# Seven products for the four blocks of the first layers, weights streamed, the low parts of the weights' four sums on VectorE

## The reference

```python
attn_out = _attn_ref(q, k, v)                       # rotate q and k, softmax(q k^T / 8) v
x = attn_out.transpose(0, 2, 1, 3).reshape(2304, 512)
h = x @ w_in;  r = np.maximum(h, 0.0);  x = (s * (r * r) + b) @ w_out              # MLP 1
h = x @ w2_in; g = h * (1.0 / (1.0 + np.exp(-1.702 * h)));  return g @ w2_out      # MLP 2
```

## Time and profile before

| what | value |
|---|---|
| runs | 1119.51, 1119.0, 1119.11 us; median 1119.11 us |
| profiled execution, span from its first to its last instruction | 1117.4 us |
| granted TensorE clock, mean | 0.998 |
| busy: PE, VectorE, ScalarE, GpSimd | 98%, 50%, 45%, 22% |
| matmuls of the first layers (L956) | 2304 of 128x384 |
| matmuls of the second layers (L984) | 1152 of 128x384, 864 of 128x512 |

### The profile page before, as it was taken

How to read it: one execution, slowest core, us unless ns; L and a number is a source line. 1 busy time by engine, 2 the same in 40 slices (tenths; PEclk the granted TensorE clock), 3 DMA queues, 4 the chain that set the end, 5 groups by cost and what they waited for, 6 DMA issues and landing times.

```text
span 1117.4 us, 16936 instructions
## 1 busy us (share of the span) xinstructions
PE 1090.4 (98%) x6522; PEld 1036.1 (93%) x6522; DVE 553.5 (50%) x885; ACT 500.8 (45%) x1031; POOL 247.4 (22%) x276
## 2 busy tenths in 40 slices
PE   4899999999999999999999999999999999999998
PEld 4899999999999999999999999999999999999997
DVE  6888888898866333333333356532332323333222
ACT  4888788878755332232332345422322222222222
POOL 6878878895720000000000000000000000000000
PEclk9999999999999999999999999999999999999999
DMA  4555454553243100000000014200000000000000
GB/s 109 126 147 145 128 152 130 147 138 91 69 132 125 37 1 1 1 1 1 1 1 1 1 57 133 76 1 1 29 1 29 1 15 15 1 29 1 29 1 29
DMA packets 59187, 59.47 MB, mean 53 GB/s; under 512 B 13780, under 2 KB 46820, under 8 KB 59108
## 3 DMA queue, kind: packets, MB, share of 16 engines
q1 hardware_dynamic: 58272, 57.90, 18.6%
q10 hardware_dynamic: 836, 0.49, 0.1%
HBM read 35.88 MB, written 4.79 MB: 36 GB/s over the span
## 4 chain that ended last, share of the span: by engine, by line
PE 90%; DVE 4%; ACT 3%; DMA 1%; issue 1%; POOL 1%; SPq 0%; ACTq 0%; POOLq 0%; DVEq 0%
PE psum L956 36%; PE psum L984 36%; PE psum L651 7%; PE psum L605 4%; PE psum L579 4%; ACT E L713 2%; DVE negmax L805 1%; PE psum L681 1%; DVE osum L835 1%; DVE Xlo L815 1%; PE psum L615 0%; PE psum L631 0%; DMA sin<-in_k_sin_dram 0%; PE psum L679 0%; DVE QK L858 0%
## 5 line engine op out<-in xcount | busy, mean ns | idle before, releaser
L956 PE MATMUL psum<-xhi,Wlo 128*128 128x384 f32 x768 | 257.8, 336 | 0.0
L956 PE MATMUL psum<-xhi,Whi 128*128 128x384 f32 x768 | 257.6, 335 | 0.0
L956 PE MATMUL psum<-xlo,Whi 128*128 128x384 f32 x768 | 257.2, 335 | 0.0
L956 PEld LDWEIGHTS psum<-xhi,Whi 128*128 128x128 f32 x768 | 144.2, 188 | 4.2
L956 PEld LDWEIGHTS psum<-xlo,Whi 128*128 128x128 f32 x768 | 144.1, 188 | 4.1
L956 PEld LDWEIGHTS psum<-xhi,Wlo 128*128 128x128 f32 x768 | 144.1, 188 | 0.0
L937 DVE SCALAR_TENSOR_TENSOR glo<-act,sb_sb,ghi 128x384 fp32r<-128x384 f32 x96 | 59.4, 619 | 145.4 <-ACT ghi L924 145.4
L924 ACT ACTIVATE ghi<-act,sb_sb 128x384 fp32r<-128x384 f32 x96 | 59.2, 617 | 157.7 <-PE psum L984 150.3
L940 DVE TENSOR_TENSOR glo<-act,ghi 128x384 fp32r<-128x384 f32 x96 | 53.6, 559 | 152.0 <-ACT ghi L926 152.0
L984 PE MATMUL psum<-ghi,Whi 128*128 128x384 f32 x384 | 128.3, 334 | 0.0
L984 PE MATMUL psum<-glo,Whi 128*128 128x384 f32 x384 | 128.3, 334 | 0.0
(11 more groups left out here) (107 smaller groups left out, 1844.4 us busy)
## 6 DMA issues: line engine op xcount, KB each, us to landing
Q<-QK SPq DMA_DIRECT2D x60, 144.0 KB, 3.1
QK<-QK SPq DMA_DIRECT2D x30, 288.0 KB, 3.4
wraw<-in_moe_w_in_dram SPq DMA_DIRECT2D x32, 256.0 KB, 2.9
wraw<-in_moe_w_out_dram SPq DMA_DIRECT2D x32, 256.0 KB, 3.1
vraw<-in_v_dram SPq DMA_DIRECT2D x32, 128.0 KB, 2.3
raw<-in_q_dram SPq DMA_DIRECT2D x30, 128.0 KB, 2.9
raw<-in_k_dram SPq DMA_DIRECT2D x30, 128.0 KB, 2.8
inv_row<-inv_dram SPq DMA_DIRECT2D x16, 144.0 KB, 2.9
```

What stands on the lines that cost most here:

```text
L956: mm = pe.matmul(hps(n), w[i][:, kt * P:(kt + 1) * P], x[C % 2][:, kt, :], start=kt == 0 and j == 0, stop=kt == KT - 1 and j == 2)
```

## The change

`H_step`, `Y_step`, `gate`, `extras`, `load_weights`, `split_w` and `first_w` are taken out. The MLPs now go by chunks of 768 tokens (3 for each MLP) and in a chunk by 8 **windows** of 256 columns of d_ff, 48 windows in all. A window's first layer is a 2 by 2 block product (two blocks of 128 d_ff columns, `a` and `b`, by two blocks of N = 384 tokens; d_model in two halves of 2 slices). It is made of 7 block products in place of 8, each of 2 slices by 3 matmuls of 128x384: `product(pe, n, k)`, k = 0 to 6. For them x has the four sums T1 to T4, made by GpSimd (`x_sum`), and the weights the four sums S1 to S4, made by GpSimd too (`w_sum`). Only two PSUM banks are there for the products: 0, 2, 4, 6 go to one, 1, 3, 5 to the other; products 0, 1 and 3 start a bank afresh, the others add to it; so ScalarE or VectorE has to read a bank out between one product and the next in it. Both layers' weights are loaded and split again in each chunk, into two buffers. The outputs of the second layer add up in the six other banks, in one set. The buffers of x are single.

What each engine issues in window n (768, 1024, ... are elements in each partition):

- PE: product 0, second layer of window n-2, block b, part 0; product 1, part 1; product 2, part 2; product 3, second layer of window n-1, block a, part 0; product 4, part 1; product 5, part 2; product 6. In MLP 1 the pieces of a block are of 512, 256, 256, 512 columns twice, in MLP 2 six of 512, with 3 matmuls each.
- ScalarE: `act_window`, VectorE: `dve_window`, GpSimd: `pool_window`, SP: the loop at the end of the diff.

```diff
-    CH = 384
+    N = 384
+    CH = 2 * N
+    W_OF = (0, 1, 4, 3, 5, 6, 2)
+    NOPS = 7
+    FRESH = (0, 1, 3)
+    POOL_OPS = 2
-    ... gate@-2 ... icp@-1 hi10@-1 hi11@-1 hi12@-1 hi13@-1 xhi@-8 split@-1 evac0@-1 ...          (ACT_ORDER)
+    ... first@-2 ... icp@-1 hi10@-1 hi11@-1 hi12@-1 hi13@-1 xc02@-1 xc03@-1 wsplit@-1 xc04@-1 evac0@-1 xc05@-1 xc06@-1 ...
-    ... lo01@0 split@-1 gate@-1 sum1@-1 ... lo13@0 max00@2 sum0@0 max01@2 ...                    (DVE_ORDER)
+    ... lo01@0 first@-1 sum1@-1 ... lo13@0 max00@2 xc02@0 xc03@0 xc04@0 sum0@0 xc05@0 xc06@0 max01@2 ...
-    POOL_ORDER = order("rot1@3 eps@0 V0@0 V1@0 vlo0@0 vlo1@0 finish@-1 xlo@-9 rot0@4")
+    POOL_ORDER = order("rot1@3 eps@0 V0@0 V1@0 vlo0@0 vlo1@0 finish@-1 rot0@4")
@@ attention_gpsimd @@
+                def first_x(k):
+                    pool.tensor_tensor(xc_hi[k][:], x_source(0, k), zero..., ALU.add).then_inc(first_x_hi, 1)
+                    pool.tensor_tensor(xc_lo[k][:], x_source(0, k), xc_hi[k][:]..., ALU.subtract).then_inc(first_x_lo, 1)
                 def after(s):
-                    first_w(pool, s, zero)
+                    if s == NPAIR - 4:
+                        for step in range(4):
+                            x_sum(pool, 0, step)
+                    if s == NPAIR - 3:
+                        first_w_sums()
+                        first_w_hi()
+                    if s == NPAIR - 2:
+                        win_low(pool, 0)
+                        first_x(0)
+                    if s == NPAIR - 1:
+                        first_x(1)
+                        w_sum(pool, 1)
@@ attention_tensor, first_H @@
-                        H_step(pe, 0)
+                        product(pe, 0, 0)
+                        product(pe, 0, 1)
@@ attention_scalar: xc is x_high (xc_hi[k], 768), wsplit is second_w (win_high(act, 1)), first is keep_first(act, 0) @@
@@ attention_vector: xc is x_low (xc_lo[k], 768), first is block_11(dve, 0) @@
+            def w_sum(pool, m):
+                pool.wait_ge(win_in[m % 2], 48 * (m // 2 + 1))
+                need(pool, win_lo_done, m)
+                need(pool, sums_lo_done, m - 1)
+                pool.tensor_tensor(S1, a21, a22, ALU.add).then_inc(w_sum_step, 1)
+                pool.tensor_tensor(S3, a11, a21, ALU.subtract)
+                pool.tensor_tensor(S2, S1, a11, ALU.subtract).then_inc(w_sum_step, 1)
+                pool.tensor_tensor(S4, a12, S2, ALU.subtract).then_inc(w_sums, 1)
+            def win_high(act, m):
+                act.wait_ge(w_sums, m + 1)
+                need(act, product_done, 7 * (m - 1))
+                act.copy(win_hi[m % 2][:, 0:3 * BLK], win_raw[m % 2][:, 0:3 * BLK])
+                act.copy(win_hi[m % 2][:, 3 * BLK:7 * BLK], wsum[:]).then_inc(win_hi_done, 1)
+            def win_low(pool, m):
+                if m == 0:
+                    sums_low(pool, m)
+                pool.tensor_tensor(win_lo[m % 2][:, 0:3 * BLK], ...[0:3 * BLK], ALU.subtract).then_inc(win_lo_done, 1)
+            def sums_low(eng, m):
+                eng.wait_ge(win_hi_done, m + 1)
+                last = eng.tensor_tensor(win_lo[m % 2][:, 3 * BLK:7 * BLK], wsum[:], win_hi[...], ALU.subtract)
+            def product(pe, n, k):
+                if k == 0:
+                    pe.wait_ge(win_lo_done, n + 1)
+                    need(pe, sums_lo_done, n)
+                if j == 0: (wait for xc_lo of product k)
+                k 0: dve_read 3n; 1: act_read 4n (MLP 2: last_read too); 2: act_read 4n+1; 3: dve_read 3n+1;
+                k 4: act_read 4n+2; 5: act_read 4n+3; 6: dve_read 3n+2
+                for t in range(HK):
+                    for i, (w, x) in enumerate(((win_hi, xc_hi), (win_hi, xc_lo), (win_lo, xc_hi))):
+                        mm = pe.matmul(hps(n, k), w[n % 2][:, at:at + P], x[k][:, t, :], ...)
+            def act_window(act, n):            (in this order; splits: last window of a chunk, evacuates: second)
+                a_b[:, 0:N] <- bank of product 6 of n-1; ga_hi <- a_a (768, waits sq_a)
+                P1 <- bank (product 0); j == 0: xc_hi[6]; splits: xc_hi[0]; win_high(act, n + 1)
+                gb_hi <- a_b (768); splits: xc_hi[1]; evacuates: bank 0
+                U2 <- bank (product 2); splits: xc_hi[2]; evacuates: banks 2, 4; wout_high(act, n) (1024)
+                P5 <- bank (product 3); splits: xc_hi[3], xc_hi[4]; a_b[:, N:] <- h_b; splits: xc_hi[5]; a_a <- h_a (768)
+            def dve_window(dve, n):
+                a_a, a_b squared or multiplied (768 each); ga_lo (768); j == 0: xc_lo[6]; splits: xc_lo[0]; evacuates: bank 1
+                block_11: h_a[:, 0:N] <- bank (product 1) + P1; sums_low(dve, n + 1) (1024)
+                gb_lo (768); evacuates: banks 3, 5; splits: xc_lo[1], [2], [3]
+                h_b[:, N:] <- bank (product 4) + P5; splits: xc_lo[4]; h_a[:, N:] <- bank (product 5) + U2; splits: xc_lo[5]
+            def pool_window(pool, n):
+                if n + 1 < WINDOWS:
+                    win_low(pool, n + 1)
+                if C + 1 < 2 * NCH and 1 <= j <= 4:
+                    x_sum(pool, C + 1, j - 1)
+                if n + 2 < WINDOWS:
+                    w_sum(pool, n + 2)
+                wout_low(pool, n)
@@ block.sync @@
+                    sp.wait_ge(pv_done, 2 * NPAIR)
+                    for n in range(WINDOWS):
+                        load_wout(sp, n)          (256 x 512 floats, one DMA; waits for wout_low of n-2)
+                        if n + 2 < WINDOWS:
+                            load_win(sp, n + 2)   (512 x 256 floats, three DMAs; waits for win_low of n)
```

More of the change, by code:

```diff
@@ new lines, in fused_kernel @@
+            sb("spare_e", [P, 256])
+            for k in range(4, NOPS):
+                xc_hi.append(sb(f"xc_hi{k}", [P, HK, N], F32R))
+                xc_lo.append(sb(f"xc_lo{k}", [P, HK, N], F32R))
+            win_hi[1] = sb("win_hi1", [P, NOPS * BLK], F32R)
+            win_lo[1] = sb("win_lo1", [P, NOPS * BLK], F32R)
+            P5 = sb("P5", [P, N])
+            sb("spare_x", [P, 640])
+            wout_hi = [sb(f"wout_hi{i}", [P, 2 * DM], F32R) for i in range(2)]
+            wout_lo = [sb(f"wout_lo{i}", [P, 2 * DM], F32R) for i in range(2)]
@@ new lines, in fused_kernel @@
+            wout_raw = [sb(f"wout_raw{i}", [P, 2 * DM]) for i in range(2)]
+            h_a, h_b = sb("h_a", [P, CH]), sb("h_b", [P, CH])
+            a_a, a_b = sb("a_a", [P, CH]), sb("a_b", [P, CH])
+            ga_hi, ga_lo, gb_hi, gb_lo = [], [], [], []
+            for i in range(2):
+                ga_hi.append(sb(f"ga_hi{i}", [P, CH], F32R))
+                ga_lo.append(sb(f"ga_lo{i}", [P, CH], F32R))
+                gb_hi.append(sb(f"gb_hi{i}", [P, CH], F32R))
+                gb_lo.append(sb(f"gb_lo{i}", [P, CH], F32R))
@@ new lines, in y_part @@
+            def y_part(pe, n, tile, part):
+                C, j = n // NJ, n % NJ
+                first, last = j == 0 and tile == 0, j == NJ - 1 and tile == 1
+                if part == 0:
+                    pe.wait_ge(wout_lo_done, n + 1)
+                    pe.wait_ge((g_lo_a, g_lo_b)[tile], n + 1)
+                gh, gl = ((ga_hi, ga_lo), (gb_hi, gb_lo))[tile]
+                gh, gl = gh[n % 2], gl[n % 2]
+                wh, wl = wout_hi[n % 2], wout_lo[n % 2]
+                pieces = [(b, 0, b, 0, BANK) for b in range(UT)] if second(n) else YT_PIECES
+                cut = (0, 2, 4, 6) if second(n) else (0, 3, 6, 8)
+                for bank, col, m, tok, size in pieces[cut[part]:cut[part + 1]]:
+                    if first and col == 0:
+                        if C == 0:
+                            freed(pe, [last_in[BANK_ORDER[2 + bank]]])
+                        else:
+                            done, value = ev_of(C - 1, bank)
+                            pe.wait_ge(done, value)
+                    for i, (w, g) in enumerate(((wh, gh), (wh, gl), (wl, gh))):
+                        if second(n):
+                            lhsT, rhs = g[:, m * P:(m + 1) * P], w[:, tile * DM:(tile + 1) * DM]
+                        else:
+                            lhsT, rhs = w[:, tile * DM + m * P:tile * DM + (m + 1) * P], g[:, tok:tok + size]
+                        mm = pe.matmul(yps(bank)[:, col:col + size], lhsT, rhs, start=first and col == 0 and i == 0, stop=last and i == 2,
+                                       skip_group_check=True)
+                    if last and col + size == BANK:
+                        mm.then_inc(y_bank, 1)
+                if part == 2 and not last:
+                    mm.then_inc((y_a, y_b)[tile], 1)
@@ L1062, in _ @@
                     attention_gpsimd(pool)
+                    for n in range(WINDOWS):
+                        pool_window(pool, n)
                 @block.tensor
```

656 lines of the change are left out of this document (391 added, 265 removed).

## The result

The changed kernel takes **1087.16 us** (median of 4 runs, 1085.56 to 1087.91) against 1119.05 for the kernel before on the same chip: a ratio of 0.9717 [0.9703, 0.9731], 32 us less. It was forecast at 1097.

A forecast was written before the change was run, and what follows sets the result against it. PE's matmul columns were taken to bound the kernel; -50.3 + 1.4 + 7.5 + 19 = -22.4 us took the span from 1117.4 to 1095.0, plus 1.7 to the median: 1097 us. Range 1076 to 1117.

The forecast's parts named there:

- the start: Behind the attention, as the MLP begins: new work stands in a row and delays PE, +19 us (6 to 27).
- rival 1: Start and chunk ends are cheap, 8 and 2 us, as turns may cost less than whole instructions: 1080 us, chance 0.22.
- the chunk ends: Last windows of chunks: 18.3 us of VectorE and GpSimd turns, 2.7 too many; five places, +7.5 us (0 to 13).
- the two small terms: MLP 1's second layer: 576 matmuls of 256 columns, +1.4 us (0 to 3); everything else in the span, 0.
- The large PE term: First layers of both MLPs: 288 matmuls of 384 columns go, -50.3 us.
- the end of PV1: Last pair's second product with V ends late, since product 1 ahead of it waits for GpSimd's split of x: +6.1 us.
- P1 +4.8: Window 0: ScalarE waits for GpSimd's w_sum(1) before copying P1, which product 2 needs: +4.8 us.
- products 2 to 6 +0.4: Window 0: products 3 to 6 have no second-layer work between them to hide the bank reads: +0.4 us.
- win_low(1) +3.6: Product 0 of window 1 waits for GpSimd's win_low(1), which stands behind `finish` of the last pair: +3.6 us.
- window 1 +3: In window 1 the P1 copy and wout_low(0), behind w_sum(2), are late once more: +3 us.
- The third: Shared SBUF reads set the pace of every window, making the kernel slower: 1158 us, chance 0.10.
- Late weights: Streamed weights arrive late and undo the gain, needing 0.47 us a window: about 1120 us, chance 0.03.

The follow-up runs named there:

- run 6: The changed kernel with GpSimd making wout_lo twice in each window, so one more instruction with two SBUF inputs: 1104.7 us, ratio 0.9878.
- run 8: The changed kernel without the low-weights-by-high-x matmul in the second slice of every first-layer product (336 matmuls): 1035.9 us, ratio 0.9263.
- run 7: The changed kernel with four GpSimd memsets of 640 elements added per window, which read nothing from SBUF: 1094.6 us, ratio 0.9789.
- run 9: run 8 with GpSimd's low parts and weight sums from weight tile 2 on replaced by memsets that read no SBUF: 1028.0 us, ratio 0.9190.
- run 1: The changed kernel with product 1 of window 0 moved behind the last pair's second product with V: 1087.6 us, ratio 0.9721.
- run 2: The changed kernel with ScalarE's wsplit, win_high of weight tile 1, moved behind the copy of P1: 1087.2 us, ratio 0.9720.
- run 3: The changed kernel with the moves of run 1 and run 2 together: 1083.6 us, ratio 0.9688.
- run 10: The changed kernel with 20 and 24 matmuls that nothing reads ahead of products 1 and 2 of window 0: 1086.0 us, ratio 0.9711.
- Run 5: The changed kernel with the low parts of the four weight sums (sums_low) back on GpSimd instead of VectorE: 1091.7 us, ratio 0.9760.
- run 12: run 4 with the split of x for product 1 moved from GpSimd to ScalarE and VectorE: 1080.9 us, ratio 0.9663.
- run 11: run 4 with VectorE's sums_low(1) behind window 0's adds into h_b and h_a, and GpSimd's win_low(1) before `finish`: 1084.5 us, ratio 0.9695.
- run 4: The changed kernel with product 1 late as in run 1, and win_high(1) behind the P5 copy of window 0: 1081.9 us, ratio 0.9672.

## Why the prediction was right, and where its sizes were off

The mechanism held: PE's columns set the time, and the cost is at the start. The time lay in the range, but 10 us below the forecast and just below the 1088 to 1104 that had a chance of 0.50; rival 1, at 1080, was 7 us off and so nearer. In spans 11.3 us were missed: 7.0 at the chunk ends, 4.2 at the start, 0.1 in the two small terms. 1.8 us of that were made up by the step from span to median, 3.5 us here and not 1.7, as the execution that was profiled was the fastest of the four: that is luck.

**Columns: right.** The large PE term is what the rows of before gave, and the small one nearly so. The windows take 15.64 and 15.71 us, with PE at work in all but 0.5 us behind 339. VectorE's adds from PSUM kept 556 ns, as said, while sums_low and gb_lo, which lie beside GpSimd's work, took 2.09 and about 2.0 us on average.

**The chunk ends: 7.5 forecast, 0.5 measured.** The step that failed is the hand layout of the last window of a chunk. Its 18.3 us of turns were to need 2.7 us more than the window has; they ran over by only 1.0 (the last split ends at 441.98), where in MLP 1 no consumer was near. Product 6 of the window before ended at about 425.3; in that window GpSimd's and then VectorE's timeline read:

```profile
429.53 2.88 POOL L1023 TENSOR_TENSOR win_lo<-win_raw,win_hi 128x768 fp32r<-128x768 f32 x1 [7.40 <-ACT win_hi L1017]
432.55 1.29 POOL L1006 TENSOR_TENSOR wsum<-win_raw 128x256 f32<-128x256 f32 x1
433.79 1.46 POOL L1007 TENSOR_TENSOR wsum<-win_raw 128x256 f32<-128x256 f32 x1
435.21 1.46 POOL L1009 TENSOR_TENSOR wsum<-wsum,win_raw 128x256 f32<-128x256 f32 x1
```

```profile
429.49 1.23 DVE L1027 TENSOR_TENSOR win_lo<-wsum,win_hi 128x1024 fp32r<-128x1024 f32 x1
430.63 2.60 DVE L1290 SCALAR_TENSOR_TENSOR gb_lo<-a_b,sb_sb,gb_hi 128x768 fp32r<-128x768 f32 x1
433.15 1.50 DVE L1167 TENSOR_TENSOR xc_lo<-xT,xc_hi 128x768 fp32r<-128x768 f32 x1
434.57 2.91 DVE L1167 TENSOR_TENSOR xc_lo<-x_sums,xc_hi 128x768 fp32r<-128x768 f32 x2
...
439.78 2.20 DVE L1167 TENSOR_TENSOR xc_lo<-xT,xc_hi 128x768 fp32r<-128x768 f32 x1 [0.31 <-ACT xc_hi L1164]
441.90 1.01 DVE L1247 SCALAR_TENSOR_TENSOR a_a<-a_a,sb_sb 128x768 f32<-128x768 f32 x1
```

Two things differ from the layout. Where both engines have work in a row, they alternate, and the starts 433.79 and 435.21 are 1.42 us apart: a sum of 0.73 and a split of 0.96 make 1.69 by whole durations, so each recorded duration holds some 0.13 us in which the other engine may already work. Part of this lies in the records, which overlap even on one engine: sums_low, 429.49 + 1.23, runs 0.09 into the next row. And the order came out kinder: win_high was ready at 4.15 behind the window's start, not 4.8, and VectorE's sums_low had its turn first (429.49), at its full speed. In the next window, which by the same measure starts at 441.0, a_a is squared by 1.9, not 4.4, and P1 is copied in time:

```profile
443.79 0.46 ACT L1122 COPY P<-psum 128x384 f32<-128x384 f32 x1
```

It ends 3.3 us into the window, needed at 5.25. The overlap of turns is worked out from this one stretch; which of the two, overlap or order, saved more was not tried.

The layout also followed the wrong consumer. In MLP 2 product 1 has to wait until VectorE has read product 6 of the window before (`last_read`), which the prediction's layout doesn't follow. That read comes behind split 5 and the product for a_a; in the first window of the last chunk but one it ends at 819.78, and product 1 starts at 819.92, 0.15 us late. With a slower first matmul behind it that is 0.23 us. It comes twice, and in run 6 the same wait takes 2.4 us, twice.

How near the limit it is, runs 6 and 8 show: 2.4 us a window more of reading costs 15 us in 48 windows, and 1.2 us a window less under PE loses 7.5.

The rule of the Trainium skill (page "SBUF — State Buffer", section "Who interferes with whom") stands with runs 6, 7 and 9: what reads costs 10 us more than what writes for the same time, and without the reads VectorE's subtract is back at 1217 ns. That one waits for the whole instruction of the other is right to within the 0.13 us above.

**The start: 19 forecast, 14.8 measured.** By steps, forecast and measured: the end of PV1 +6.1, +6.6 (PV0, forecast 1.5 late, came in time, since eps was 1.5 us earlier than laid out); P1 +4.8, +1.8; products 2 to 6 +0.4, +1.7; win_low(1) +3.6, +1.5; window 1 +3, +3.2. Another +1 was forecast for the clock, at no place. So the order of the places was right, and GpSimd's row of work was shorter than laid out: w_sum(1) ended at 318.2, not 320.3. The 6.6 agree with the 6.1 by luck: the wait is 4.2 of them, and 2.4 are product 1 and PV1 at the lower clock. With products 2 to 6 that makes 4.1 us at the lower clock, where 1 was forecast; the waits alone are 10.7 us against 18.

**What the forecast did not see is that these terms don't add up.** "6.1 late" reads as if product 1 behind PV1 were worth 6 us; run 1 shows it is worth nothing by itself, and run 2 the same for wsplit. The two delays lay side by side between w_sum(1) and P1, and only run 3 shortened both. Likewise the clock: 4.1 us are seen in front of window 1, and run 10 got back at most 1.2.

**The titled part.** The forecast said that moving sums_low frees only the difference of two prices on the shared reads, 1.2 us a window. Run 5 says 4.5 us in all for undoing it, since most of that difference fits into the windows' slack.

**The rivals.** The first (start 8, chunk ends 2) was nearly right on the chunk ends; its start was 6.8 too low, the forecast's 4.2 too high. The third, slower by shared reads, names a mechanism that is there: it did not decide because adds and copies from PSUM do lie beside GpSimd's reads, as its "against" had it: the add into h_b at 437.40 takes 0.54 us beside GpSimd's sum from 436.75 to 438.08. Late weights: no sign of it. What stays open is the rest of the start, 7.6 us in run 12: waits for h_b 2.2, h_a 2.0 and wout_lo 1.1, and a clock of 0.57 in 324 to 328.

## What to carry to other kernels

Where PE is full, price a change in columns first, then check each helper's load against the window, and the time that VectorE's two-SBUF-input operations and GpSimd's instructions need together, for they take turns; work with an input in PSUM is free of that. A full budget of turns need not cost anything if no consumer is near, so follow every consumer with little slack, each bank that has to be read out too, rather than add the turns up. At the start of a phase list what stands in each engine's order in front of the first results: undoing one of two delays that lie side by side gains nothing, so try them together before you call one harmless.

## What had not been expected of the hardware

- Turns on the shared reads are shorter than the recorded durations by some 0.13 us (1.42 us for a pair of 0.73 and 0.96). Moving two operations to other turns put first ya 3.1 us later (run 11 against run 4).
- Memsets on GpSimd, which read no SBUF, still cost 7.5 us (run 7), more than half of it in the steady part.
- The clock fell to 0.50 behind a wait of 4.05 us and again to 0.61 around 326 us behind one of 1.7; matmuls that nothing reads held it at 1.00 up to 328, but it fell behind the next wait, of 2.20 us, for next to no gain.
